# Two attention heads per block turned into one: halves of keys and queries turned step by step, and scores from 64x64 products, in a fused attention and MLP kernel

## What is computed

```python
# q, k, v: (2, 8, 768, 64) float32; block 32, window 16
k_sum = k.reshape(B, H, nb, block, D).max(axis=3)      # 24 summary keys
v_sum = v.reshape(B, H, nb, block, D).mean(axis=3)     # 24 summary values
scores_l = scale * q @ k.T, masked to |i - j| < 16
scores_s = scale * q @ k_sum.T + log(32)
a = softmax over [scores_l, scores_s]                  # exp, sum + 1e-9
out = a @ [v, v_sum]
```

## Time and profile before

| | before |
|---|---|
| median of 3 runs | 491.66 us (491.5 to 492.65) |
| the profiled execution's own time | 489.64 us |
| its span, first to last instruction | 487.9 us |
| mean granted TensorE clock | 0.996 |
| PE busy, ACT busy, DVE busy, POOL busy | 467.0, 227.4, 296.9, 150.9 us |

### The profile page before, as it was taken

One profiled execution on the slowest core, in us unless ns is written; L12 is line 12 of the kernel. 1 busy time (PEld: TensorE's weight loads), 2 busy tenths in 40 slices (PEclk: granted clock), 3 DMA queues, 4 the chain that ended last, 5 costly groups with the idle time before them and its releaser, 6 DMA issues.

```text
span 487.9 us, 7908 instructions
## 1 busy us (share of the span) xinstructions
PE 467.0 (96%) x2896; PEld 419.9 (86%) x2896; DVE 296.9 (61%) x672; ACT 227.4 (47%) x475; POOL 150.9 (31%) x155
## 2 busy tenths in 40 slices
PE   5789898999999999999999999999999999999996
PEld 4677776788999999999999999899899889989985
DVE  5789996479666665557545875666636346354511
ACT  3999995554442333413332433355544335244411
POOL 7646774260256335653326544000000000000000
PEclk9999998999999999999999999999999999999999
DMA  9999944300121212122103315310010010001001
GB/s 210 236 228 235 205 101 70 130 12 32 45 89 43 87 50 80 60 70 86 44 14 117 113 60 173 111 63 0 1 64 1 0 43 21 0 0 64 0 0 64
DMA packets 42235, 36.92 MB, mean 76 GB/s; under 512 B 20704, under 2 KB 34528, under 8 KB 42208
## 3 DMA queue, kind: packets, MB, share of 16 engines
q1 hardware_dynamic: 42208, 36.58, 27.1%
HBM read 33.43 MB, written 3.15 MB: 75 GB/s over the span
## 4 chain that ended last, share of the span: by engine, by line
PE 84%; issue 4%; ACT 4%; DVE 4%; POOL 2%; DMA 1%; ACTq 0%; DVEq 0%; POOLq 0%
PE bank L1220 19%; PE bank L1222 19%; PE bank L1221 19%; PE bank L1353 14%; PE bank L1354 7%; PE bank L1202 2%; PE bank L1272 1%; ACT e_sb L630 1%; PE bank L1168 1%; ACT qbd L610 1%; PE bank L1250 1%; DVE s_sb L868 1%; POOL xL L541 1%; DMA kn<-in_k_dram 1%; ACT kt L618 1%
## 5 line engine op out<-in xcount | busy, mean ns | idle before, releaser
L1220 PE MATMUL bank<-ucH,w1H 128*128 128x384 f32 x168 | 56.8, 338 | 0.0
L1222 PE MATMUL bank<-ucH,w1L 128*128 128x384 f32 x168 | 56.5, 336 | 0.0
L1221 PE MATMUL bank<-ucL,w1H 128*128 128x384 f32 x168 | 56.4, 336 | 0.0
L754 ACT ACTIVATE rH<-c 128x384 fp32r<-128x384 f32 x36 | 18.9, 526 | 68.6 <-DVE c L1065 68.6
L1222 PE MATMUL bank<-xkH,WkL 128*128 128x384 f32 x128 | 43.1, 336 | 0.0
L1220 PE MATMUL bank<-xkH,WkH 128*128 128x384 f32 x128 | 43.0, 336 | 0.0
L1221 PE MATMUL bank<-xkL,WkH 128*128 128x384 f32 x128 | 42.9, 335 | 0.0
L1141 DVE SCALAR_TENSOR_TENSOR k<-bank,kr 128x384 f32<-128x384 f32 x32 | 17.8, 556 | 33.4 <-ACT kr L804 33.4
L582 POOL TENSOR_TENSOR w2L<-stg,w2H 128x512 fp32r<-128x512 f32 x24 | 37.6, 1586 | 1.0
L1222 PE MATMUL bank<-WvH,k2L 128*128 128x512 f32 x96 | 37.8, 394 | 0.0
L1221 PE MATMUL bank<-WvL,k2H 128*128 128x512 f32 x96 | 37.8, 394 | 0.0
(11 more groups left out here) (142 smaller groups left out, 1209.0 us busy)
## 6 DMA issues: line engine op xcount, KB each, us to landing
stg<-in_moe_w_ch_dram SPq DMA_DIRECT2D x24, 512.0 KB, 3.4
vw<-in_v_dram SPq DMA_DIRECT2D x16, 240.0 KB, 4.3
kn<-in_k_dram SPq DMA_DIRECT2D x8, 384.0 KB, 4.5
qn<-in_q_dram SPq DMA_DIRECT2D x8, 384.0 KB, 5.5
v<-in_v_dram SPq DMA_DIRECT2D x8, 384.0 KB, 4.1
out_dram<-o_sb SPq DMA_DIRECT2D x12, 256.0 KB, 2.0
stg<-in_moe_w_k_dram SPq DMA_DIRECT2D x4, 512.0 KB, 3.4
stg<-in_moe_w_v_dram SPq DMA_DIRECT2D x4, 512.0 KB, 4.0
```

The costliest lines, as they stand in the source:

```text
L754: act.activation(rH[slot][:, f, half * GR:half * GR + GR], src, ACT.Relu).then_inc(rh_done, 1)
L1220: pe.matmul(dst, wH, mH, start=start, stop=False, **more)
L1221: pe.matmul(dst, wH, mL, start=False, stop=False, **more)
L1222: return pe.matmul(dst, wL, mH, start=False, stop=stop, **more)
```

## The change

A block is now two units of one head: 128 queries of head h, since query and key of one head lie in 64 partitions of `qT` and `kt`. Neither `qbd` nor `kw` exists any more: the keys are read in place. For a pair of blocks (one per head), four products of 64 x 64 x 96 (two units by two heads, each in its own quarter of the array) write the local columns, and two products of 64 x 128 x 24 write the summary columns. The outputs of the two heads go to two different banks out of three. `kt` and `ks` are double. A row of constants 1e-9 and ones in `vw` and `aT` adds the 1e-9 inside the AV product, so that the row sums' own instruction goes away.

The DVE step is: maxima, then at r = 0 both DVE copies of head 0's keys, at r = 1 both of head 1's, at r = 2 the summary keys and the cast. ACT turns out no keys after the opening, queries of one head at r = 1 and of the other at r = 2, and does the whole split of `u` one pair later. On PE a half is turned per place: `turn_k` h0 before and h1 after the scores at r = 0, `turn_q` before the scores at r = 1 and at r = 2; the sum of values moves to r = 0. The loop over pairs is unrolled. In the opening the constants go to DVE and POOL in another order, and pair 1 is turned between the first scores. The weights `w_tok1` are split before `w_tok2`.

```diff
+        def score_bank(r, n):
+            return bS[(2 * r + n % 2) % 3]
...
-            for par in range(2):
-                dve.memset(qbd[par][:, :, :], 0.0).then_inc(init_dve, 1)
...
+            for par in range(2):
+                dve.memset(vw[par][0:LOC, 0, :, 0:D], 0.0).then_inc(vw_ready, 1)
+                dve.memset(vw[par][0:LOC, NU - 1, :, 0:D], 0.0).then_inc(vw_ready, 1)
+                dve.memset(vw[par][0:LOC, :, :, D:D + 1], 1.0).then_inc(vw_ready, 1)
+                dve.memset(vw[par][LOC:COLS + 1, :, :, 0:D], 0.0)
+                dve.memset(vw[par][LOC:COLS + 1, :, :, D:D + 1], 1e-9).then_inc(vw_ready, 1)
...
+            def turn_out_k(pp, par, h, free):
+                dve.wait_ge(k_turned, 2 * pp + h + 1)
...
+                for j in range(2):
+                    dve.tensor_copy(kt[par][h * D:h * D + D, WIN + j:WIN + S:2],
+                                    (bK, bQ)[h][j * D:j * D + D, 0:NB * P]).then_inc(kt_written, 1)
...
-            def cut_windows(par, free):
-                dve.tensor_copy(kw[par][:, :, 0:LOC], windows).then_inc(kw_ready, 1)
...
                     if p < NP - 1:
-                        maxima(G + 3, r, 1 - gp, GU * G + GU)
+                        maxima(G + 3, r, GU * G + GU)
...
-                    row_sums(G, r, gp)
-                    if prep and r == 0:
-                        turn_out_k(p + 2, 0, 2 * p + 4)
...
+                    if prep and r < 2:
+                        turn_out_k(p + 2, par, r, 3 * p + 3)
+                    elif prep:
+                        summary_keys(p + 2, par)
+                    if r == NG - 1 and 1 <= p <= NWT:
                         high_wt(p - 1)
-                    invert(G, r)
+                    invert(G, r, gp)
                     normalise(G, p, r, gp)
...
-                for n in range(GU):
-                    t = GU * r + n
-                    ins = pe.matmul(bS[gp][:, COLS * n:COLS * n + COLS], qbd[par][:, t, :], kw[par][:, t, :],
-                                    start=True, stop=True)
+                for n in range(0, GU, 2):
+                    c0, two = COLS * (n // 2), 2 * r + n // 2
+                    for e in range(2):
+                        q0, t = e * UQ, 2 * two + e
+                        for h in range(2):
+                            pe.matmul(score_bank(r, n + (h + e) % 2)[q0:q0 + UQ, c0:c0 + LOC],
+                                      qT[par][ROWS[(h + e) % 2], t * UQ:t * UQ + UQ],
+                                      kt[par][ROWS[(h + e) % 2], t * UQ:t * UQ + LOC], start=True, stop=True)
+                    for h in range(2):
+                        ins = pe.matmul(score_bank(r, n + h)[:, c0 + LOC:c0 + COLS],
+                                        qT[par][ROWS[h], two * P:two * P + P], ks[par][ROWS[h], :],
+                                        start=True, stop=True)
                 ins.then_inc(scores_done, 1)
...
+            pe.wait_ge(kt_written, 4)
+            for h in range(2):
+                turn_k(1, 1, h, (bK, bQ)[h])
+            scores(0, 0, 0, None)
...
-                        pe.wait_ge(wl_done, NWT)
+                        pe.wait_ge(wl_done, NWT // 2 + 1)
...
+                    if r == 0 and p + 1 < NP:
+                        pe.wait_ge(q_written, 4 * p + 8)
+                        pe.wait_ge(vs_read, p + 1)
+                        sum_vs(p + 1)
+                        if prep:
+                            pe.wait_ge(kt_written, 4 * p + 8)
+                            turn_k(p + 2, par, 0, bK)
+                    elif prep:
+                        pe.wait_ge(kt_written, 4 * p + 8 + 2 * r)
+                        turn_q(p + 2, par, r - 1, (bK, bQ)[r - 1])
+                    if p < NP - 1:
+                        scores(p + 1, 1 - par, r, GU * (G + 2) + 2)
                     if prep and r == 0:
-                        turn_k(p + 2, par, 8 * (p - par) + 32, 5 * (p + 2))
-                    if prep and r == 1:
-                        turn_q(p + 2, par, 8 * (p - par) + 32)
+                        pe.wait_ge(vs_read, p + 2)
+                        turn_k(p + 2, par, 1, bQ)
```

More of the change, by code:

```diff
@@ L130, in build_program @@
         e_sb = [reg.take(f"e_sb{i}", [P, GU, COLS]) for i in range(2)]
-        aT = [reg.take(f"aT{i}", [COLS, GU, P]) for i in range(2)]
+        aT = [reg.take(f"aT{i}", [COLS + 1, GU, P]) for i in range(2)]
         reg = Region(R0, RS)
@@ L557, in _ @@
                 pair(p, p % 2)
+            split_x(NP - 1)
             def sums_w1(n):
@@ L668, in pair, with high_x @@
                         high_h1(0)
[L669 to L691 removed]
+                    if r == 0 and p >= 1:
+                        high_x(p - 1)
+                    if prep and r >= 1:
+                        turn_out_q(p + 2, par, r - 1, (bK, bQ)[r - 1])
+            def high_x(p):
+                act.wait_ge(norm_done, NG * p + NG + 2)
+                act.activation(x_halves(xH, p), x_of(p), ACT.Copy).then_inc(xh_done, 1)
+            for p in range(NP):
+                pair(p, p % 2, p < NP - 2)
+            high_x(NP - 1)
             def high_w1(n):
@@ new lines, in _, with turn_out_q @@
+            dve.memset(u[:, :, :, 0:1], 0.0).then_inc(init_dve, 1)
+            def turn_out_q(pp, par, h, bank_q):
+                dve.wait_ge(q_turned, 2 * pp + h + 1)
+                for j in range(2):
+                    dve.tensor_scalar(qT[par][h * D:h * D + D, j:S:2], bank_q[j * D:j * D + D, 0:NB * P],
+                                      float(D) ** -0.5, None, ALU.mult).then_inc(q_written, 1)
+            def turn_out_k(pp, par, h, free):
+                dve.wait_ge(k_turned, 2 * pp + h + 1)
+                if free is not None and h == 0:
+                    dve.wait_ge(scores_done, free)
+                for j in range(2):
+                    dve.tensor_copy(kt[par][h * D:h * D + D, WIN + j:WIN + S:2],
+                                    (bK, bQ)[h][j * D:j * D + D, 0:NB * P]).then_inc(kt_written, 1)
@@ L1169, in turn @@
                 return ins
-            def turn_k(pp, par, loaded, free):
-                pe.wait_ge(ld_k[par], loaded)
-                if free is not None:
-                    pe.wait_ge(qbank_read, free)
-                for h in range(2):
-                    turn(kn[par][:, h, :, :], (bK, bQ)[h]).then_inc(k_turned, 1)
-            def turn_q(pp, par, loaded, banks=(bQ, bK), free=True):
-                pe.wait_ge(ld_q[par], loaded)
-                if free:
-                    pe.wait_ge(kt_written, 4 * pp + 4)
-                for h in range(2):
-                    turn(qn[par][:, h, :, :], banks[h]).then_inc(q_turned, 1)
@@ new lines, in scores @@
+                ins.then_inc(scores_done, 1)
+            pe.wait_ge(ident_ready, 1)
+            for h in range(2):
+                turn_k(0, 0, h, (bK, bQ)[h])
+            for h in range(2):
+                turn_q(0, 0, h, bA[h])
+            pe.wait_ge(kt_written, 4)
+            for h in range(2):
+                turn_k(1, 1, h, (bK, bQ)[h])
+            scores(0, 0, 0, None)
+            for h in range(2):
+                turn_q(1, 1, h, bA[h])
+            scores(0, 0, 1, 2)
+            pe.wait_ge(sel_ready, 1)
@@ L1218, in three @@
+            pe.wait_ge(kt_written, 8)
+            sum_vs(0)
+            scores(0, 0, 2, GU + 2)
             def three(dst, wH, wL, mH, mL, start, stop, **more):
```

291 lines of the change are left out of this document (115 added, 176 removed).

## The result

The changed kernel takes 521.7 us (median of 4 runs, 518.1 to 533.9), the kernel before 491.9 beside it: 1.058 times, 95% interval 1.051 to 1.065. The prediction was 501.1 with a range of 486 to 516. The direction was right, the size three times too small.

A forecast was written before the change was run, and what follows sets the result against it. PE bounds everything behind the attention; inside it the changed kernel is bound by the PE-DVE circle. Step 18 +11.6, pair 6 -3.06 + 0.90: +9.4 us on the profiled 489.64, 499.1, plus 2.0 for the median: 501.1, range 486 to 516.

The forecast's parts named there:

- The price of the scores (S = 1.34): PE's score products per step: 1.34 us instead of 0.89, including four more tile shape switches at 0.15 each.
- The circle: Turn, scores, maxima, copies, next turn between PE and DVE: 3.89 us per step, a pair 11.14 us against 9.46.
- cold: Rival: PE idles about 1 us each step, clock halves, S + 0.33 more per step, over 515; 0.10 together with serial.
- serial: Rival: row halves of the array don't overlap in the scores, S = 2.1, +25, 517; 0.10 together with cold.
- The sum: All terms to the end of the attention and pair 6: -18.7 + 21S = +9.4 us.
- The opening: Start to step 0: pair 1's keys turned ahead of the first scores; AV of step 0 at 22.4 us, before 20.84.
- the product that I had at 20.0: Opening, PE: the summed values' product, placed at 20.0 us when POOL's three sums end.
- Pair 6: Transposes 18 to 19: 4.14 us instead of 7.20, a gain of 3.06, no wait for POOL's weight split.
- The two steps behind it: Pair 6's two later steps, bound by PE: each pays S - 0.89 = 0.45 us more.

The follow-up runs named there:

- grouped: The changed kernel with all eight 64x64 score products of a step first, then the four 64x128 summary products; 510.9 us.
- Keys first: The changed kernel with DVE's copies of turned keys, and the summary keys at r = 2, ahead of the maxima; 497.6 us, 1.012 times before.
- The run with one wait more: The kernel before, with AV of each step of pairs 0 to 5 waiting on PE for the four maxima of the scores just made; 499.8 us, 1.019.
- fill, full array: The changed kernel with six full-array identity transposes added behind the exponentials' transposes in every step of pairs 1 to 5; 513.6 us, 1.047.
- the combined kernel: The changed kernel with keys copied ahead of the maxima, scores regrouped, and full-array transposes in both gaps of the opening; 490.0 us, 1.001.

## Why the prediction was wrong

**The price of the scores (S = 1.34) was right:** 1.32 measured; and its parts, since taking two changes of shape away saves 0.27 where the sum said 0.30. That row halves run side by side, which no row showed, is so: in "grouped" 16 records of 64x64x96 take 0.49 us to the next start, where at the rate of the rows before (0.11 us for 120 columns, so 0.09 for 96) one behind the other would take 1.4 and two at once 0.7.

**The circle was right in kind and 7% short.** 4.18 us from one waiting turn to the next (51.35 to 55.53) where 3.89 was worked out: the half turn takes 0.47 to the scores' start (51.35 to 51.82), not 0.33; 0.26 pass until the maxima, 0.93 until the copies begin (54.33 on DVE) and 1.20 to the turn. A pair 11.65 instead of 11.14 makes 2.6 us over five pairs. Keys first shows that the circle was the bound: 9.64.

**The step that failed is the clock, set aside in the rival "cold",** which was given less than 0.10 together with "serial": "PE idles about 1 us in each step and the clock falls to its half level". The sum took the full clock for every step, at no cost. The rival's mechanism happened; against it I had set that PE was busy 5.49 of 8 us at a clock of 1.00. That reading was weak twice. The kernel before has its first entry of the granted clock at 13.3 us, so that the 1.00 of this stretch from 12 to 20 us is not a granted level in its first 1.3 us; and its products are mostly on the full array. The run with one wait more shows that such rows keep the clock at 25% idle; the changed kernel lost it at 14% with scores on quarters of the array. The row gave the idle share without the kind of work. Cost: 13.0 us in the pairs, 3 in pair 6, and a part of the opening that was not measured apart. Why the level fell at 55.6 and 72.6 and not before, and hardly at all in "grouped", stays open.

**The opening.** I had AV of step 0 at 22.4 us; it came at 26.00. The sum was right in its order, but the scores and turns ran at half speed up to 28.2: the scores of step 3 take 2.16 instead of 1.32, and from the summed values' product (21.63) to the transposes of step 1 (27.07) it is 5.44 us:

```profile
21.63 0.62 PE L1158 MATMUL bank<-v,sel 96*24 96x128 f32 x2 [1.28 <-DVE qT L838]
...
23.01 0.60 PE L1174 MATMUL bank<-kt,qT 64*64 64x96 f32 x8
...
26.00 1.14 PE L1261 MATMUL bank<-vw,aT 121*64 121x65 f32 x16
```

Before, full speed began at 13.3, and the prediction took it for granted from the maxima of the opening on. Not all of the 3.6 us is the clock: the product that I had at 20.0 started at 21.63, by the profile behind DVE's copies of the second pair's queries, which the sum did not have. Step 3 is 7.3 us late; the sum, taken to this point, has 20.75 + S + 2 x (2.55 + S) + 0.67 = 30.5 for the 27.32 before, 3.2 late. How much of the difference is the clock and how much the later first loads and sums was not taken apart; with the full clock for most of the opening, and two changes of shape less in each step, the combined kernel has step 3 at 28.29, 1.0 behind before.

**Pair 6.** Predicted 4.14 from step 18 to 19, measured 7.68: all at the half level (it ends at 113.6). In kernels that had the full clock it is 4.57 with the keys first, 4.98 with the circle closed ("fill, full array", where PE waits 0.47 for the summary keys) and 3.81 in the kernel before with this part alone. So the term was 0.4 to 0.8 too good with the new scores, and the gain real. The two steps behind it took 3.41 each (3.29 predicted).

With the clock at full the changed kernel's span would have been, by these terms, 522.0 - 13.0 in the pairs - some 3 in pair 6 (7.68 to 4.57 or 4.98) - some 4 in the opening = 502, 504 as a time. That is an estimate that no run shows; its 4 come from step 3 at 30 to 31 us, where the sum had it, and so take the whole loss there for the clock's. The range of 486 to 516 holds 504. The range did not reach 522 because the cold rival (S + 0.33 on each step, "over 515") was left outside it on account of its small chance. What it would add to a step was right: S + 0.33 is 1.67, and a pair at the half level takes 5.1 more than one at full, 1.7 a step.
